# Scores of a gated linear attention on four quarters of TensorE, r and k scaled in one operation, score banks filled in bursts of two

## Chip, cores and metric

One core of one Trainium2 chip. The time is the device's, in microseconds, median of three runs.

## What is computed

Inputs r, k, v, w are [4, 8, 768, 48] (batch, head, token, feature), u is [8, 48]. The attention is a recurrence with a decay for each feature; its output, 3,072 rows of 384, goes through two feed-forward blocks.

```
for t in range(S):
    cur = einsum('bhd,bhe->bhde', u * k[t], v[t])
    y[t] = einsum('bhd,bhde->bhe', r[t], state + cur)
    state = w[t][..., None] * state + einsum('bhd,bhe->bhde', k[t], v[t])
h = maximum(maximum(x @ w1, x @ w2), x @ w3);  x = h @ w_out          # [3072, 384]
h = x @ w_in2;  solu = h * softmax(h);  ln = layernorm(solu) * g_ln;  out = ln @ w_out2
```

## The kernel before

**Groups and slots.** Tokens are cut into 6 units of 128. A group `g` is one unit of one batch element, 24 in all; its 8 heads lie in 4 pairs `q`, the first head of a pair on partitions 0 to 47 and the second on 64 to 111. Within a group the scores of token s against token t are made by levels, since the decay between two tokens is a product: level 0 takes a token with itself (with `u`), level 1 its neighbour, and the levels L = 2 to 64 take, in each block of 2L tokens, the late half (r) against the early half (k). Before each next level r of the late half and k of the early half are multiplied in place by products of w, a tree of products that GpSimd makes (`tree`, L411). A group has 8 such slots, `s` = 0 to 7, so 192 in all.

**One slot on each engine.** TensorE (`scores`, L439) makes 4 matmuls, one a pair, of 112 rows (both heads), 128 weight columns (tokens s) and 128 moving columns (2 heads x 64 tokens t). The heads are kept apart by `r_own`, which holds r twice, each time with zeros where the other head's features are. The result fills one PSUM bank. VectorE (`scores`, L700, and `scale`, L685) scales k (L696) and r (L698) for the next level, and for `s` up to 4 moves the slot's result through a mask to `scoresT` (L711, or L719 as a predicated copy). For `s` = 5 to 7 ScalarE copies blocks (L601). ScalarE's `base` (L576) makes `r_base` and `k_base` with `u` for slots 0 and 1 (L583 to L588).

**The mix** `M` of a group (TensorE, L462) turns k to tokens (L471), multiplies the carried state (L483, L484) and the values by the scores (L486), into columns 0 to 63 and 64 to 111 of the output, and makes the update of the state (L493). `v` is VectorE's new state, `q` and `p` split y and regroup it by DMA (`y_last` to `xT`).

**Feed-forward work.** `u` are 9 matmuls of 512 columns (L498 to L500), `d` the same, `l` 18, `t` 8 transposes (L552), `o` 8 fp32 matmuls of 384 columns, 16 records (L561). `e`, `x`, `c`, `n`, `w` are the softmax and norm on ScalarE and VectorE; `z` splits a chunk of weights.

**What sets the order.** Every engine walks the same list `PROGRAM`, put together from plans written out by hand (`START`, `FIRST`, `STEADY` four times, `LAST`); a dot stands for the next slot in `slot_order`, where slots 4 to 7 of a group alternate with slots 0 to 3 of the next, a digit for the next slot of that group. SP walks it too and issues the loads. The score banks are 4 and 5 (`LEV`), used in turn by slots and by the mix's turned k and update. TensorE waits in `wait_drained` for the reader of the bank's user two places back, so one slot's matmuls run while the other bank is read:

```
n = BANK_AT[user] - 2
kind, task = BANK_USERS[n]
...
if task[1] < 2 + MASKED:
    return masked, MASKED_AT["s", task]
return score_copied, COPIED_AT["s", task]
```

A slot also waits for the scaling of the slot before in its own group (`scaled`), VectorE's scaling for the end of that slot's matmuls (`scored`).

Of the kernel before, what the change touches and what calls it, by code (L numbers as in the profile page):

```python
# [22 lines left out]
UPDATES = 7  # L23
RING_K, RING_W, RING_P = 3, 2, 2
# [22 lines left out]
def splits(chunks, on_pool):  # L47
# [12 lines left out]
    . . . . u00 z u01 z u02 z u10 u11 u12 u20 u21 d0 . u22 d1 u30 d2 z . u31 . . M v z z . z u32 u40 u41 . u42 . d3 .  # L60
    u50 p . z u51 u52 . . d4 q d5 z M p . e0 v l0 g . x0 l1 q c0 . e1 t0 g . c1 x1 g . n00 g l2 . t1 n01 . e2 . n02 o0
    n03 M w0 e3 c2 v x2 l3 . w1 o1 . . t2 p . x3 . o2 n10 c3 q . . t3 . . M w2 p n11 n12 n13 q w3 o3 v"""

STEADY = """
    . . u00 . u01 . u02 u10 u11 d0 u12 . . u20 u21 . u22 . d1 v u30 u31 M d2 u32 . u40 u41 . . u42 u50 d3 . . u51 . .
    u52 d4 q . d5 M l0 v x0 . l1 . e0 c0 . t0 . e1 x1 . q c1 n00 o0 . . n01 t1 p . v M n02 w0 n03 . l2 p . q e2 x2 e3
    l3 c2 . o1 w1 t2 . . x3 p . n10 o2 c3 n11 t3 . p n12 w2 n13 . M q w3 v o3"""
# [63 lines left out]
COPIED_AT = places(lambda t: t[0] == "s" and t[1][1] >= 2 + MASKED)  # L131
UPDATED = places(lambda t: t[0] == "s" and t[1][1] >= 1)


def attention_moe_kernel(nc, r_in, k_in, w_in, v, u_in, w1, w2, w3, w_out, w_in2, w_out2, g_ln, base_mask, level_mask, ident_in, out):
# [3 lines left out]
    with ctx:  # L139
# [12 lines left out]
        base_m = sb("base_m", [128, 2, C // 2])  # L152
        level_m = sb("level_m", [128, MASKED, C // 2], u32)
        ident = sb("ident", [128, 128])

        r_own = sb("r_own", [128, RING_K, 2, PAIRS * C])
        k_sb = sb("k_sb", [128, RING_K, PAIRS * C])
# [5 lines left out]
        r_base = sb("r_base", [128, 2, PAIRS, C // 2])  # L163
        scoresT = sb("scoresT", [128, RING_P, PAIRS, 2, C])
# [25 lines left out]
        LEV = [4, 5]  # L190
        Y, OUT = 6, 7

        cleared = [sem(f"cleared{i}") for i in range(2)]
# [7 lines left out]
        kr_loaded = [sem(f"kr_loaded{i}") for i in range(RING_K)]  # L201
# [5 lines left out]
        k_scaled = sem("k_scaled")  # L207
# [84 lines left out]
        def logits_of(m, t):  # L292
# [3 lines left out]
        BANK_USERS = [("s", n) if kind == "s" else (part, n) for kind, n in PROGRAM  # L296
                      for part in (("s",) if kind == "s" else ("kt", "upd") if kind == "M" else ())] + [("after", 0), ("after", 1)]
        BANK_AT = {user: n for n, user in enumerate(BANK_USERS)}

        def bank_of(user):  # L300
            return LEV[BANK_AT[user] % 2]

        def drained(user):

            n = BANK_AT[user] - 2
            if n < 0:
                return None
            kind, task = BANK_USERS[n]
            if kind == "kt":
                return k_copied, task[0] + 1  # L310
            if kind == "upd":
                return state_new, task[0] + 1
            if task[1] < 2 + MASKED:
                return masked, MASKED_AT["s", task]
            return score_copied, COPIED_AT["s", task]

# [3 lines left out]
        def _(sp):  # L320
# [7 lines left out]
            def load_kr(g):  # L328
                slot = g % RING_K
                if g >= RING_K:  # L330
                    sp.wait_ge(y_done, g - RING_K + 1)
                    sp.wait_ge(k_turned, g - RING_K + 1)
                sp.dma_start(k_sb[0:PR, slot, :], k_in[g]).then_inc(kr_loaded[slot], 16)
                if g < RING_K:
                    sp.wait_ge(cleared[0], slot + 1)
                    sp.wait_ge(cleared[1], slot + 1)
                sp.dma_start(r_own[0:D, slot, 0, :], r_in[g, 0]).then_inc(kr_loaded[slot], 16)
                sp.dma_start(r_own[HB:PR, slot, 1, :], r_in[g, 1]).then_inc(kr_loaded[slot], 16)
# [67 lines left out]
        def _(pool):  # L406
            for i in range(RING_K):
                nc.gpsimd.memset(r_own[0:HB, i, 1, :], 0.0).then_inc(cleared[1], 1)
            nc.gpsimd.memset(state[:], 0.0).then_inc(cleared[1], 1)
# [22 lines left out]
        def _(pe):  # L432

            def wait_drained(user):
                before = drained(user)
                if before:
                    pe.wait_ge(before[0], before[1])

            def scores(g, s):  # L439
                slot = g % RING_K  # L440
                bank = ps[:, bank_of(("s", (g, s))), :]
                wait_drained(("s", (g, s)))
                if s == 0:
                    pe.wait_ge(r_base_done, g + 1)
                elif s == 1:
                    pe.wait_ge(k_base_done, g + 1)
                else:
                    pe.wait_ge(scaled, UPDATED["s", (g, s - 1)])
                for q in range(PAIRS):
                    cols = slice(q * C, (q + 1) * C)  # L450
                    r = r_own[0:PR, slot, :, cols]
                    if s == 0:
                        stationary, moving = k_sb[0:PR, slot, cols], r_base[0:PR, :, q, :]
                    elif s == 1:
                        stationary, moving = k_base[0:PR, cols], r.rearrange("p i (t e) -> p i t e", e=2)[:, :, :, 1]
                    else:
                        stationary = k_sb[0:PR, slot, cols]
                        moving = r.rearrange("p i (n h l) -> p i n h l", h=2, l=LEVELS[s - 2])[:, :, :, 1, :]
                    last = nc.tensor.matmul(bank[:, cols], stationary, moving, start=True, stop=True)  # L459
                last.then_inc(scored, 1)  # L460

            def mix(g):  # L462
                b, slot, p = g % B, g % RING_K, g % RING_P
                kt, upd, yp = ps[:, bank_of(("kt", (g,))), :], ps[:, bank_of(("upd", (g,))), :], ps[:, Y, :]
                wait_drained(("kt", (g,)))
                if g == 0:
                    pe.wait_ge(c_loaded, 16 * 3)
                    pe.wait_ge(cleared[1], RING_K + 1)
                pe.wait_ge(k_scaled, UPDATED["s", (g, SLOTS - 1)])
# [3 lines left out]
                pe.wait_ge(scaled, UPDATED["s", (g, SLOTS - 1)])  # L473
# [5 lines left out]
                if g >= B:  # L479
                    pe.wait_ge(state_new, g - B + 1)  # L480
                for q in range(PAIRS):
                    cols = slice(q * C, (q + 1) * C)
                    nc.tensor.matmul(yp[0:HB, cols], state[0:PR, b, q, 0:HB], r_own[0:PR, slot, 0, cols], start=True, stop=False)  # L483
                    nc.tensor.matmul(yp[HB:PR, cols], state[0:PR, b, q, 0:D], r_own[0:PR, slot, 1, cols], start=True, stop=False)  # L484
                    for i in range(2):
                        last = nc.tensor.matmul(yp[i * HB:i * HB + D, cols], v_sb[:, slot, (2 * q + i) * D:(2 * q + i + 1) * D],  # L486
                                                scoresT[:, p, q, i, :], start=False, stop=True)
                last.then_inc(y_done, 1)
                wait_drained(("upd", (g,)))
# [30 lines left out]
            def up(m, j, w):  # L520
                n = 3 * j + w
                if n == 0:
                    wait_split(3 * KD)
                    pe.wait_ge(repacked, B * REPACK * (m + 1))
                if n >= 2:
# [7 lines left out]
            def logits_(m, t):  # L533
# [4 lines left out]
                if m == UNITS - 1 and t == 2:  # L538
                    for before in map(drained, (("after", 0), ("after", 1))):
                        pe.wait_ge(before[0], before[1])  # L540
# [26 lines left out]
        def _(act):  # L567
# [8 lines left out]
            def base(g):  # L576
                slot = g % RING_K
                act.wait_ge(kr_loaded[slot], 48 * (g // RING_K + 1))
                if g:
                    act.wait_ge(scored, SCORED["s", (g - 1, 1)])  # L580
                r_even = r_own[0:PR, slot, :, :].rearrange("p i (q t e) -> p q i t e", q=PAIRS, e=2)[:, :, :, :, 0]
                for q in range(PAIRS):
                    last = nc.scalar.activation(r_base[0:PR, :, q, :], r_even[:, q, :, :], ACT.Copy, scale=u_sb[0:PR, q:q + 1])  # L583
# [7 lines left out]
            def scores(g, s):  # L591
# [3 lines left out]
                bank = ps[:, bank_of(("s", (g, s))), :].rearrange("p (a n l) -> p a n l", a=2 * PAIRS, l=L)  # L595
                dst = scoresT[:, g % RING_P, :, :, :].rearrange("p q i (n h l) -> p (q i) n h l", h=2, l=L)
                act.wait_ge(masked, MASKED_AT["s", (g, 1 + MASKED)])
                act.wait_ge(scored, SCORED["s", (g, s)])
                for n in range(C // (2 * L)):
                    early = slice(n * 2 * L, n * 2 * L + L)  # L600
                    last = nc.scalar.copy(dst[early, :, n, 1, :], bank[early, :, n, :])  # L601
                last.then_inc(score_copied, 1)

            def mix(g):
# [3 lines left out]
                nc.scalar.copy(k_tok[:].rearrange("p q d -> p (q d)"), ps[:, bank_of(("kt", (g,))), 0:PAIRS * PR]).then_inc(k_copied, 1)  # L608
# [71 lines left out]
        def _(dve):  # L680
            for i in range(RING_K):
                nc.vector.memset(r_own[0:PR, i, 0, :], 0.0).then_inc(cleared[0], 1)
            dve.wait_ge(c_loaded, 16 * 3)

            def scale(g, n):  # L685
# [3 lines left out]
                dv = decay_of(g, n).rearrange("p (n h) -> p n h", h=2)  # L689
# [5 lines left out]
                early = halves(k_sb[0:PR, slot, :], L)[:, :, 0, :]  # L695
# [157 lines left out]
```

## Time and profile before

| | |
|---|---|
| median of 3 runs | 858.72 us (857.13 to 861.47) |
| profiled execution | 861.66 us |
| its span | 859.9 us |
| mean granted TensorE clock | 0.99 |
| TensorE busy, records | 815.1 us, 5088 matmuls |
| VectorE / ScalarE / GpSimd busy | 473.9 / 331.4 / 76.2 us |
| first `u` of the six units | 91.5, 226.2, 361.3, 496.3, 631.4, 760.0 us |

An fp32 matmul shows as two records, each with its weight load (PEld). Records of matmuls overlap, since a record reaches to the end of the pipeline: the distance of starts is the pace, the duration is not. Forms such as `112*128 112x128` give weight rows x weight columns, then rows x moving columns. "Idle before" is the engine's idle time just before the instructions of a group.

### The profile page before, as it was taken

The page shows a single profiled execution, that of the slowest core. Times are in us where ns is not written, and L with a number is a line of the kernel's source. Part 1 is how long each engine was busy: PE and PEld are TensorE (multiplying, and loading weights), DVE is VectorE, ACT ScalarE, POOL GpSimd, SP SyncE. Part 2 cuts the span into 40 slices and gives each one's busy share as a digit, 9 for nine tenths or more (in the row PEclk, how much of TensorE's full clock was granted, in tenths as well). Part 3 has the DMA queues.
Part 4 walks back from the last instruction along what each step waited for, and adds up shares of the span by engine and source line. Part 5 has one row for each costly group of instructions (what it writes and reads, how often), then busy time and mean ns, then how long its engine had stood idle before and what let it go on. Part 6 is the DMA issues. An engine that isn't in the chain of part 4 may idle for free.

```text
span 859.9 us, 13390 instructions
## 1 busy us (share of the span) xinstructions
PE 815.1 (95%) x5088; PEld 669.9 (78%) x5088; DVE 473.9 (55%) x958; ACT 331.4 (39%) x741; POOL 76.2 (9%) x181
## 2 busy tenths in 40 slices
PE   5778999999999999999999999999999999999997
PEld 5667788887788887788887688887778888778774
DVE  4977556766543685544666544666644467412241
ACT  4444232566231365321463422344613235511153
POOL 3221111110010110100101101001101010000000
PEclk9988999999999999999999999999999999999999
DMA  8452201020101102201011011011020100000000
GB/s 221 123 170 62 65 26 53 6 83 26 63 1 40 44 8 63 62 3 41 1 45 55 20 57 42 1 45 55 15 63 1 41 6 11 19 23 1 1 10 27
DMA packets 27824, 36.50 MB, mean 42 GB/s; under 512 B 5232, under 2 KB 18160, under 8 KB 27760
## 3 DMA queue, kind: packets, MB, share of 16 engines
q1 hardware_dynamic: 27200, 35.41, 13.7%
q8 instruction: 41, 0.67, 0.3%
q10 hardware_dynamic: 560, 0.23, 0.1%
q14 instruction: 23, 0.19, 0.1%
HBM read 28.55 MB, written 4.72 MB: 39 GB/s over the span
## 4 chain that ended last, share of the span: by engine, by line
PE 87%; DVE 9%; issue 2%; ACT 1%; DMA 1%; SPq 0%; ACTq 0%; DVEq 0%
PE ps L459 19%; PE ps L498 16%; PE ps L500 15%; PE ps L499 15%; PE ps L561 14%; DVE r_own L698 3%; DVE scoresT L719 2%; PE ps L552 2%; PE ps L486 2%; PE ps L493 1%; DVE k_sb L696 1%; PE ps L484 1%; PE ps L471 1%; DVE scoresT L711 1%; PE ps L483 1%
## 5 line engine op out<-in xcount | busy, mean ns | idle before, releaser
L459 PE MATMUL ps<-r_own,k_sb 112*128 112x128 f32 x1152 | 159.2, 286 | 20.7 <-DVE r_own L698 11.8
L459 PEld LDWEIGHTS ps<-r_own,k_sb 112*128 112x128 f32 x1152 | 149.4, 198 | 33.1 <-issue 11.1
L498 PE MATMUL ps<-xT,w_moe 128*128 128x512 f32 x324 | 131.7, 406 | 1.5 <-DMA xT<-y_last 0.9
L561 PE MATMUL ps<-w_moe_out,zT 128*128 128x384 f32 x384 | 128.6, 488 | 3.9 <-ACT out_sb L674 2.6
L499 PE MATMUL ps<-xT,w_moe 128*128 128x512 f32 x324 | 127.9, 395 | 0.0
L500 PE MATMUL ps<-xT,w_moe 128*128 128x512 f32 x324 | 127.8, 395 | 0.0
L561 PEld LDWEIGHTS ps<-w_moe_out,zT 128*128 128x128 f32 x384 | 71.0, 190 | 50.0 <-issue 3.5
L698 DVE TENSOR_TENSOR r_own<-r_own,decay 112x512 f32<-112x512 f32 x144 | 103.2, 717 | 0.0
L696 DVE TENSOR_TENSOR k_sb<-k_sb,decay 112x256 f32<-112x256 f32 x144 | 62.6, 435 | 71.8 <-PE ps L459 71.5
L601 ACT COPY scoresT<-ps 16x128 f32<-16x128 f32 (+2 forms) x168 | 55.9, 333 | 95.9 <-PE ps L459 94.6
L639 ACT CAST h_x<-e_sb 128x512 fp32r<-128x512 f32 x36 | 22.3, 620 | 155.7 <-DVE e_sb L755 147.9
L498 PEld LDWEIGHTS ps<-xT,w_moe 128*128 128x128 f32 x324 | 61.1, 189 | 14.9 <-issue 1.4
L500 PEld LDWEIGHTS ps<-xT,w_moe 128*128 128x128 f32 x324 | 61.0, 188 | 14.3
L499 PEld LDWEIGHTS ps<-xT,w_moe 128*128 128x128 f32 x324 | 61.1, 189 | 12.3
L421 POOL TENSOR_TENSOR decay<-w_sb 112x256 f32<-112x256 f32 x24 | 15.4, 641 | 567.0 <-issue 537.1
L719 DVE COPY_PREDICATED scoresT<-level_m,ps 128x512 f32<-128x512 uint32 x72 | 65.0, 903 | 0.0
L498 PE MATMUL ps<-w_moe,h_x 128*128 128x512 f32 x144 | 58.8, 409 | 1.5 <-DVE h_x L764 1.5
L500 PE MATMUL ps<-w_moe,h_x 128*128 128x512 f32 x144 | 56.8, 395 | 0.0
L755 DVE TENSOR_TENSOR e_sb<-ps,e_sb 128x512 f32<-128x512 f32 x36 | 24.9, 691 | 57.8 <-PE ps L500 57.7
L499 PE MATMUL ps<-w_moe,h_x 128*128 128x512 f32 x144 | 56.8, 394 | 0.0
L749 DVE TENSOR_TENSOR e_sb<-ps,e_sb 128x512 f32<-128x512 f32 x36 | 24.9, 691 | 49.3 <-PE ps L500 49.3
L768 DVE TENSOR_REDUCE neg_max<-ps 128x1 f32<-128x1024 f32 x24 | 29.3, 1221 | 40.5 <-PE ps L500 40.5
(82 smaller groups left out, 1210.3 us busy)
## 6 DMA issues: line engine op xcount, KB each, us to landing
k_sb<-in_k SPq DMA_DIRECT2D x24, 224.0 KB, 2.7
w_sb<-in_w SPq DMA_DIRECT2D x24, 224.0 KB, 3.5
r_own<-in_r SPq DMA_DIRECT2D x48, 96.0 KB, 3.2
v_sb<-in_v SPq DMA_DIRECT2D x24, 192.0 KB, 3.7
out<-out_sb SPq DMA_DIRECT2D x24, 192.0 KB, 1.9
xT<-y_last SPq DMA_DIRECT2D x144, 16.0 KB, 1.9
e_sb<-in_w SPq DMA_DIRECT2D x5, 384.0 KB, 3.4
zT<-in_w SPq DMA_DIRECT2D x4, 384.0 KB, 5.4
```

The costliest lines, as they stand in the source:

```text
L459: last = nc.tensor.matmul(bank[:, cols], stationary, moving, start=True, stop=True)
L498: nc.tensor.matmul(o, a[0], b[0], start=first, stop=False)
L499: nc.tensor.matmul(o, a[0], b[1], start=False, stop=False)
L500: return nc.tensor.matmul(o, a[1], b[0], start=False, stop=last)
L561: last = nc.tensor.matmul(ps[:, OUT, 0:DM], zT[:, t % 2, c, :], w_moe2_out[:, c, :], start=(c == 0), stop=(c == J2 - 1))
L601: last = nc.scalar.copy(dst[early, :, n, 1, :], bank[early, :, n, :])
L696: nc.vector.tensor_tensor(early, early, dv[:, :, 1].unsqueeze(2).to_broadcast([PR, blocks, L]), ALU.mult).then_inc(k_scaled, 1)
L698: nc.vector.tensor_tensor(late, late, dv[:, :, 0].unsqueeze(1).unsqueeze(3).to_broadcast([PR, 2, blocks, L]), ALU.mult).then_inc(scaled, 1)
L719: nc.vector.copy_predicated(dst, mk, src).then_inc(masked, 1)
L749: nc.vector.tensor_tensor(c1, ps[:, (3 * j + 1) % 2, :], c1, ALU.max).then_inc(c2_done, 1)
L755: nc.vector.tensor_tensor(h_max, ps[:, (3 * j + 2) % 2, :], c1, ALU.max).then_inc(c3_done, 1)
L768: nc.vector.tensor_reduce(neg_max[:, t:t + 1], logits_of(m, t), AX.X, ALU.max, negate=True).then_inc(max_done, 1)
```

## The change

Scores go to four quarters of the array: `i`, the head, picks 48 rows, `h`, the half of the tokens, 64 weight columns. r is held once, beside k in `rk_sb`, loaded by one DMA. The head's result goes to a bank of its own, so a slot needs two banks and fills 128 columns of each, and two slots, a burst, fill the first half of both (`at` is the place). Up to two slots that follow each other on TensorE form a burst; its first slot waits for the readers of the last burst in these banks, and masks and copies wait for the burst's last matmul. Before the first `u`, bursts alternate between banks 4, 5 and 0, 1 (`EARLY`). One operation scales r and k. A mask is two operations, one for each half of the tokens. `r_base` is made for one copy of r. The state's products use one head's 48 rows each and stand ahead of all products with the values. The plans `START`, `FIRST` and `STEADY` are new, `LAST` is not.

```diff
-    b0 0 a0 0 a1 0 z 1 1 0 1 0 a2 z 0 1 0 1 z 0 z 1 b1 z M z v p q 1 2 2 1 2 z b2 v M a3 z 3 p 2 q 2 z 2 3 2 2 3 M b3 v
-    q b4 3 3 a4 3 p 4 3 4 3 4 a5 M v q 4 p b5"""
+    0 a0 0 1 0 1 a1 0 z b0 1 0 z a2 0 1 b1 0 1 z 0 1 z v M q p 1 2 1 2 z 2 b2 a3 b3 z M v p z z 3 2 2 3 z q 2 a4 3 2 3
+    2 M v p b4 q 3 4 3 p 4 3 4 3 M v q a5 4 b5"""
...
+    . . u00 . . u01 u02 u10 u11 u12 . . u20 v u21 M d0 . u22 u30 u31 d1 . . d2 u32 u40 u41 . d3 u42 . u50 . . u51 u52 .
+    d4 q d5 M v l0 . x0 e0 . p q c0 l1 . p . e1 t0 . . o0 x1 . . n00 p n01 n02 c1 l2 n03 v t1 M o1 w0 q . w1 x2 e2 . c2
+    l3 . t2 . e3 . x3 c3 n10 o2 . n11 . . t3 w2 n12 M n13 q v o3 p w3 . ."""
...
+def bursts():
+
+    found, begun = [], False
+    for n, (kind, task) in enumerate(t for t in PROGRAM if t[0] in "sMudlto"):
+        begun = begun or kind == "u"
+        if kind == "s":
+            if found and found[-1][0][-1][0] == n - 1 and len(found[-1][0]) < 2:
+                found[-1][0].append((n, task))
+            else:
+                found.append(([(n, task)], begun))
+    return [([task for _, task in slots], begun) for slots, begun in found]
...
+                BANK_USERS["s", n] = LEV if n % 2 == 0 or BURSTS[n][1] else EARLY
...
-                wait_drained(("s", (g, s)))
+                banks, at, begins = banks_of(g, s)
+                if begins:
+                    wait_drained(("s", BURST_OF[g, s][0]))
...
-                    last = nc.tensor.matmul(bank[:, cols], stationary, moving, start=True, stop=True)
+                    for h in range(2 if s < SLOTS - 1 else 1):
+                        for i, rows in enumerate((slice(0, D), slice(HB, PR))):
+                            early = slice(q * C + h * HALF, q * C + (h + 1) * HALF)
...
+                                stationary, moving, width = k_sb[rows, slot, early], r_sb[rows, slot, q * C + HALF:(q + 1) * C], HALF
+                            last = nc.tensor.matmul(ps[h * HALF:(h + 1) * HALF, banks[i], at + q * width:at + (q + 1) * width],
+                                                    stationary, moving, start=True, stop=True)
...
-                    nc.tensor.matmul(yp[0:HB, cols], state[0:PR, b, q, 0:HB], r_own[0:PR, slot, 0, cols], start=True, stop=False)
-                    nc.tensor.matmul(yp[HB:PR, cols], state[0:PR, b, q, 0:D], r_own[0:PR, slot, 1, cols], start=True, stop=False)
+                    for i, rows in enumerate((HB, D)):
+                        part = slice(i * HB, i * HB + D)
+                        nc.tensor.matmul(yp[i * HB:i * HB + rows, cols], state[part, b, q, 0:rows], r_sb[part, slot, cols],
+                                         start=q == 0, stop=False, skip_group_check=True)
...
-                nc.vector.tensor_tensor(early, early, dv[:, :, 1].unsqueeze(2).to_broadcast([PR, blocks, L]), ALU.mult).then_inc(k_scaled, 1)
-                late = r_own[0:PR, slot, :, :].rearrange("p i (n h l) -> p i n h l", h=2, l=L)[:, :, :, 1, :]
-                nc.vector.tensor_tensor(late, late, dv[:, :, 0].unsqueeze(1).unsqueeze(3).to_broadcast([PR, 2, blocks, L]), ALU.mult).then_inc(scaled, 1)
+                row = rk_sb[0:PR, slot, :, :]
+                both = bass.AP(row.tensor, row.offset + L, [row.ap[0], [PAIRS * C - L, 2], [2 * L, blocks], [1, L]])
+                by = decay_of(g, n).rearrange("p (n h) -> p h n", h=2).unsqueeze(3).to_broadcast([PR, 2, blocks, L])
+                nc.vector.tensor_tensor(both, both, by, ALU.mult).then_inc(scaled, 1)
...
+                for h in range(2):
+                    rows = slice(h * HALF, (h + 1) * HALF)
+                    src, dst = score_views(g, s, rows)
```

## Rows read from the trace of the kernel before

**Rows 1.** The page: busy time of each engine; the chain by engine.

```profile
PE 815.1 (95%) x5088; PEld 669.9 (78%) x5088; DVE 473.9 (55%) x958; ACT 331.4 (39%) x741; POOL 76.2 (9%) x181
...
PE 87%; DVE 9%; issue 2%; ACT 1%; DMA 1%; SPq 0%; ACTq 0%; DVEq 0%
```

**Rows 2.** Busy time by stretch: stretch, length, engines, clock, DMA share, GB/s.

```profile
0.00:91.40 91.40, 65.97 (x527) 60.38 (x528) 67.59 (x120) 37.69 (x106) 20.71 (x50) 0.91 0.49 141
91.40:226.10 134.70, 131.52 (x834) 107.81 (x834) 79.97 (x158) 60.90 (x135) 18.52 (x33) 1.00 0.13 40
226.10:361.20 135.10, 132.68 (x851) 109.47 (x850) 76.39 (x158) 52.37 (x119) 10.55 (x28) 1.00 0.12 35
...
631.30:759.90 128.60, 127.12 (x803) 104.00 (x801) 68.96 (x146) 47.48 (x101) 5.36 (x14) 1.00 0.08 22
```

**Rows 3.** TensorE's waits, first 91.4 us: total, times, longest.

```profile
PE ps L459 <- DVE r_own L698: 11.8, 8, 1.9
```

**Rows 4.** Timeline of TensorE, two slots: start, length, records.

```profile
304.34 1.05 PE L459 MATMUL ps<-r_base,k_sb 112*128 112x128 f32 x8
305.24 1.06 PE L459 MATMUL ps<-r_own,k_sb 112*128 112x128 f32 x8
```

**Rows 5.** Timeline of TensorE, state products of a mix.

```profile
319.33 0.27 PE L484 MATMUL ps<-r_own,state 112*48 112x128 f32 x1
319.34 0.27 PE L483 MATMUL ps<-r_own,state 112*64 112x128 f32 x1
319.44 0.27 PE L484 MATMUL ps<-r_own,state 112*48 112x128 f32 x1
```

**Rows 6.** Its update and the score behind it; the update's group by form.

```profile
320.75 0.67 PE L493 MATMUL ps<-v_sb,k_tok 128*64 128x48 f32 x16
321.35 0.38 PE L459 MATMUL ps<-r_own,k_sb 112*128 112x128 f32 x1
...
L493 PE MATMUL ps<-v_sb,k_tok 128*64 128x48 f32 x192 | 15.4, 223 | 4.6 <-DVE scoresT L719 4.1 <-ACT k_tok L608 0.4
```

**Rows 7.** Timeline of TensorE from the transposes to the state products.

```profile
318.37 0.55 PE L471 MATMUL ps<-ident,k_sb 112*128 112x112 f32 x4
...
318.66 0.26 PE L471 MATMUL ps<-ident,k_sb 112*128 112x112 f32 x1
...
318.85 0.32 PE L483 MATMUL ps<-r_own,state 112*64 112x128 f32 x1
...
319.01 0.27 PE L483 MATMUL ps<-r_own,state 112*64 112x128 f32 x1
```

**Rows 8.** Timeline of TensorE, full-width matmuls behind another update.

```profile
189.07 0.50 PE L498 MATMUL ps<-w_moe,h_x 128*128 128x512 f32 x1
189.40 0.39 PE L499 MATMUL ps<-w_moe,h_x 128*128 128x512 f32 x1
189.63 0.39 PE L500 MATMUL ps<-w_moe,h_x 128*128 128x512 f32 x1
```

**Rows 9.** Timeline of VectorE, two stretches: scaling and masks.

```profile
30.62 0.43 DVE L696 TENSOR_TENSOR k_sb<-k_sb,decay 112x256 f32<-112x256 f32 x1 [0.21 <-PE ps L459]
30.96 0.68 DVE L698 TENSOR_TENSOR r_own<-r_own,decay 112x512 f32<-112x512 f32 x1
31.57 0.69 DVE L719 COPY_PREDICATED scoresT<-level_m,ps 128x512 f32<-128x512 uint32 x1
32.16 0.95 DVE L743 TENSOR_TENSOR w_moe<-zT,w_moe 128x768 fp32r<-128x768 f32 x1
...
121.70 1.31 DVE L719 COPY_PREDICATED scoresT<-level_m,ps 128x512 f32<-128x512 uint32 x1
```

**Rows 10.** ScalarE's `r_base` by form: busy us, mean ns, idle before.

```profile
L583 ACT ACTIVATE r_base<-r_own,u_sb 112x128 f32<-112x128 f32 x96 | 31.4, 399 | 11.4 <-PE ps L459 7.1 <-DMA r_own<-in_r 3.9
```

**Rows 11.** DMA issues: KB each, us to landing.

```profile
r_own<-in_r SPq DMA_DIRECT2D x48, 96.0 KB, 3.2
```

**Rows 12.** TensorE's group of scores from 91.4 us on, by form.

```profile
L459 PE MATMUL ps<-r_own,k_sb 112*128 112x128 f32 x928 | 121.4, 276 | 5.3 <-DVE scoresT L719 2.8 <-DVE scoresT L711 2.5
```

More of the change, by code:

```diff
@@ L190, in attention_moe_kernel @@
         LEV = [4, 5]
+        EARLY = [0, 1]
         Y, OUT = 6, 7
-        cleared = [sem(f"cleared{i}") for i in range(2)]
+        cleared = sem("cleared")
         u_loaded = sem("u_loaded")
@@ L200, in attention_moe_kernel @@
         wg_ready = sem("wg_ready")
[L201 removed]
+        rk_loaded = [sem(f"rk_loaded{i}") for i in range(RING_K)]
         v_loaded = [sem(f"v_loaded{i}") for i in range(RING_K)]
@@ L293, in logits_of @@
             return ps[:, pair_of(m, t):pair_of(m, t) + 2, :].rearrange("p a n -> p (a n)")
[L296 to L301, printed above, removed]
-        def drained(user):
[L305 to L315, printed above, removed]
+        BANK_USERS = {}
@@ new lines, in attention_moe_kernel @@
+        for kind, task in PROGRAM:
+            if kind == "s" and BURST_OF[task][1] == 0:
+                n = BURST_OF[task][0]
+                BANK_USERS["s", n] = LEV if n % 2 == 0 or BURSTS[n][1] else EARLY
+            elif kind == "M":
+                BANK_USERS["kt", task[0]] = LEV[:1]
+                BANK_USERS["upd", task[0]] = LEV[1:]
+            elif kind == "u" and task in ((0, 0, 0), (0, 0, 1)):
+                BANK_USERS[kind, task[2]] = EARLY[task[2]:task[2] + 1]
+        BANK_USERS["after", 0] = LEV
@@ new lines, in drained, with banks_of @@
+        def drained(user):
+            users = list(BANK_USERS)
+            before = users[:users.index(user)]
+            found = {}
+            for bank in BANK_USERS[user]:
+                for other in [o for o in before if bank in BANK_USERS[o]][-1:]:
+                    for signal, value in read_out(other):
+                        found[signal.name] = (signal, value)
+            return list(found.values())
+        def banks_of(g, s):
+            n, place = BURST_OF[g, s]
+            return BANK_USERS["s", n], place * 2 * C, place == 0
@@ new lines, in score_views, with score_ready @@
+        def score_views(g, s, rows):
+            banks, at, _ = banks_of(g, s)
+            width = HALF if s == SLOTS - 1 else HALF // 2
+            src = ps[rows, banks[0]:banks[0] + 2, at:at + PAIRS * width].rearrange("p i (q t) -> p i q t", t=width)
+            return src, scoresT[rows, g % RING_P, :, :, :]
+        def score_ready(g, s, engine):
+            n, place = BURST_OF[g, s]
+            slots = BURSTS[n][0]
+            other = [t for t in slots[:place] if (t[1] < 2 + MASKED) != engine]
+            return SCORED["s", slots[-1]], other[-1:]
@@ L332, in load_kr @@
                     sp.wait_ge(k_turned, g - RING_K + 1)
[L333 to L338, printed above, removed]
+                sp.dma_start(rk_sb[0:PR, slot, :, :], rk_in[g]).then_inc(rk_loaded[slot], 16)
             def load_v(g):
@@ L406, in _ @@
         def _(pool):
-            for i in range(RING_K):
-                nc.gpsimd.memset(r_own[0:HB, i, 1, :], 0.0).then_inc(cleared[1], 1)
-            nc.gpsimd.memset(state[:], 0.0).then_inc(cleared[1], 1)
+            nc.gpsimd.memset(state[:], 0.0).then_inc(cleared, 1)
             def tree(g):
@@ L538, in logits_ @@
                 if m == UNITS - 1 and t == 2:
-                    for before in map(drained, (("after", 0), ("after", 1))):
-                        pe.wait_ge(before[0], before[1])
+                    wait_drained(("after", 0))
                 for n in range(2):
@@ L680, in _ @@
         def _(dve):
-            for i in range(RING_K):
-                nc.vector.memset(r_own[0:PR, i, 0, :], 0.0).then_inc(cleared[0], 1)
+            nc.vector.memset(scoresT[HB:128, :, :, :, 0:HALF], 0.0).then_inc(cleared, 1)
             dve.wait_ge(c_loaded, 16 * 3)
@@ L721, in y_low @@
+                last.then_inc(masked, 1)
             def y_low(g):
```

157 lines of the change are left out of this document (88 added, 69 removed).

## The prediction

> **What bounds the kernel now.** I read the page's busy shares and its chain of waits first. TensorE is busy for 95% of the span and holds 87% of the chain; VectorE holds 9% of it at 55% busy [rows 1]. Then the stretches: in the first 91 us TensorE is busy for only 66 of 91.4 us at a mean clock of 0.91, and VectorE for 68 [rows 2]. From 91.4 to 760 us TensorE idles for 2.4 to 3.2 us in each unit of some 135 us, and 1.5 in the last of them (length less busy time, [rows 2]). So there are two regimes: a start bound by the dependent steps between TensorE and VectorE, where the scores' matmuls wait 11.8 us on the scaling of `r_own` alone [rows 3], and a rest in which TensorE's own work is the time.
>
> **What a slot costs.** The 192 slots are 4 fp32 matmuls each, which the trace shows as 8 records; two slots start 0.90 us apart, so 0.112 us a record [rows 4]. Of the 192, 40 stand ahead of the first `u` in `START` and 152 behind it.
>
> **Part 1: scores on quarters.** A slot becomes 16 matmuls (8 for the last level), 32 records, with 64 weight columns and 32 moving columns (64 in the last level). No row shows a matmul on 48 rows of one half. The nearest rows are the ones that already use column halves. The state products on output columns 0 to 63 and 64 to 111 start 10 ns apart, and the next pair 0.11 us later [rows 5]: the column halves run side by side, each at the pace that a full-width record has. The update's 16 records of 48 moving and 64 or 48 weight columns take 0.67 us; less the 0.22 us of the last one, the eighth of a half starts 0.45 us after the first, 0.064 us a record, a first delayed one among them [rows 6]. That is a little over half of 0.112 for half the weight columns, though the moving columns fell to 48: loading weights sets the pace. I take 0.06 us a record. With four quarters side by side, each has 8 records a slot (4 pairs, two records each): 8 x 0.06 = 0.48 us; in the last level two quarters have 8 records each, again 0.48. The bounds: if only column halves overlap, 16 x 0.06 = 0.96 (if all parts share the pace of the update's 16 records in 0.45 us, 32 x 0.028 = 0.90); if a record costs its 32 moving columns alone, a quarter of 0.112, 8 x 0.028 = 0.22. I take 0.48, since a quarter's records have the update's weight columns. After `START` that is 152 x (0.90 - 0.48) = 63 us less.
>
> The Trainium skill, TensorEngine Tiling (Array Packing), Instruction Overhead, speaks against this: it gives each matmul some 60 cycles of overhead and says not to tile a dimension that is already small. At 2.4 GHz that would be, as an estimate from that page, 25 ns for each of 32 records or 0.8 us a slot, and part 1 would shrink to 15 us. By that page the change would gain nothing here; what it says hangs on whether parts share the overhead, and the 10 ns between two column halves [rows 5] speak against that.
>
> **Part 2: changing the array's division.** Each run of slots between other work now goes from whole array to quarters and back. The trace shows both ways, where the mix does it. Into halves: the last of four transposes starts at 318.66 (the first at 318.37, so 0.096 apart), the first state product at 318.85, 0.19 later, so +0.09; its second pair comes 0.15 us later where 0.11 is the rule, +0.04 [rows 7]. Back: the last update record starts at 321.20 and the next score at 321.35, +0.09 over a pace of 0.06; and the second full-width matmul behind such a change comes 0.33 us after the first, where 0.23 is the rule, +0.10 [rows 6, 8]: its weights were not loaded ahead. Together 0.33 us a round. I counted the new plans: 85 runs of slots behind `START` that are not joined to a mix, so 28 us, and the mix, which now goes from quarters (state products) to column halves (values), one more change of 0.09 in 20 groups, 2 us. Sum +30. Bounds for a round: 0.10, if weights can be loaded ahead after all, and 0.50.
>
> **Part 3: VectorE.** The scaling of k (0.43 us) disappears and r and k, 512 elements a partition as `r_own` had, take one operation. Back to back, operations start 0.34 us (256 elements) and 0.61 us (512) after each other [rows 9]. A mask becomes two operations of 64 partitions and 256 elements: 2 x 0.34 for 0.59 to 0.61, +0.08; the first level, at 1.31 where the next ones take 0.69 [rows 9], perhaps +0.15. After `START` VectorE has room: 80 of 135 us busy [rows 2]. In `START` it is on the path: 34 scalings less 0.34 each are 11.6 us, 26 masks give 2 back, and the slots' shorter matmuls are mostly eaten by the coarser waits of part 4. I take -9 us. ScalarE's `r_base` halves its elements, from 399 ns [rows 10] to less, off the path. r comes with k in one transfer of 448 KB for three of 416 KB in all, of which r's took 3.2 us each [rows 11], asked for a group or more ahead; SP issues two fewer a group and no longer waits for the zeroed `r_own`, and the first load may land some tenths of a us later or earlier. Nothing.
>
> **Part 4: one set of banks.** Before, a slot waited for the one two places earlier; now both slots of a burst fill both banks, and a burst waits until VectorE and ScalarE have read both slots of the last one. Behind the waiting matmul the whole of TensorE queues. After a burst ends VectorE owes the second slot's scaling (0.61) and four mask operations (4 x 0.34), with a hop of 0.1 some 2.1 us. One `u` between bursts (9 x 0.23 = 2.1 us, [rows 8]) covers that. I walked the new order for places with less cover behind `START`: 8 where two bursts adjoin, 11 with only a set of transposes (0.88 us) between. 8 x 2.1 + 11 x 1.2 = 30 us. Of today's waits of scores behind `START`, 5.3 us [rows 12], these take the place: +25.
>
> **Sum.** -63 + 30 - 9 + 25 = -17 us. The profiled execution took 861.7 us (span 859.9), 3 us over the median of 858.7 of the runs shown; 861.7 - 17 = 845 for a profiled one, and 842 for the median.
>
> **Rivals.**
> A, the quarters don't run side by side, so that the change doesn't do what it says: the row halves share what loads weights, or all quarters share one pace of records. No row has two row halves at once. A slot then takes 0.90 to 0.96 us; at 0.96 the 152 slots add 9 instead of taking 63, the changes keep their 30, `START` gains only some 5, and the uncovered places shrink to perhaps +10, as VectorE works under longer slots: 859 + 9 + 30 - 5 + 10 = 903 us, at 0.90 some 894. It decides the sign from about 0.60 us a slot on. For it: the update's pace is set by weights. Against it: column halves load side by side [rows 5], and rows of the array are fed by partitions of their own. The Trainium skill, TensorEngine Tiling, Key Properties, says that different tiles load and multiply in parallel; no row of this case shows it for row halves. Chance 0.12, all slower.
> B, the single set of banks eats the gain. If the need after a burst is 3.0 us, not 2.1 (masks on half the partitions at nearly their old 0.69, the first level at 1.3 twice), the 19 places add 0.9 each, 17 us, and places covered by one `u` begin to wait. 859 to 866 us. For it: VectorE's waits already lead in `START` [rows 3]. Against it: 256 elements take 0.34 us back to back, 0.43 alone [rows 9]. Chance 0.14, of which 0.10 within the bound and 0.04 slower.
> C, changing the division costs 0.10 a round, since another quarter's weights can be loaded while one runs: 85 x 0.23 = 20 us less, 822 us. Against it: two changes that each show theirs [rows 6 to 8]. Chance 0.10, faster.
> D, TensorE works so little in the start that its clock falls. It is at 0.91 there already with 66 of 91 us busy [rows 2], and the change takes off some 16 us of that work. At half clock a slot of 0.48 takes 0.96; if 30 of the 40 do, and half of it shows, 7 us: 849. Chance 0.04, faster.
>
> **Numbers.** The forecast itself gets 0.60, between 830 and 853 us: 0.58 faster, 0.01 no change and 0.01 slower. A measurement of this kernel tells 0.5%, 4.3 us, from no change. Faster: 0.58 + 0.10 + 0.04 = 0.72. Same: 0.01 + 0.10 = 0.11. Slower: 0.01 + 0.12 + 0.04 = 0.17. The range, 814 to 867, holds the forecast, B, D and all but the end of C, and leaves out A and what lies under C: about 0.16.
>
> **What would show it.** Right: a slot of `L459`'s successor spans about 0.48 us and two slots under 1.1; 64-column records of one quarter start 0.06 us apart and four quarters within 0.03; the first full-width matmul after a burst shows a gap of about 0.1 to the next; waits of scores on VectorE's masks of some 2 us, four a unit; a unit of about 133 us where 135.1 stood; the first `u` at about 82 us, not 91. Wrong: records one after the other at 0.028 or more (A), a unit over 135 us with waits at places that have a `u` between (B), no gap at the changes (C), PEclk under 0.8 before 80 us (D).

## The result and the profile after

The changed kernel takes 861.43 us against 858.07 in runs side by side, a ratio of 1.0034 (95% interval 1.0020 to 1.0049): 0.3% slower where 1.9% faster was forecast. (One of its 20 executions took 2567 us, and one of the ten of run h1 below 4246 us; both are left out of the ratios.) The time lies near the upper end of the range of 814 to 867, on the other side of the kernel before.

The page of the changed kernel, busy time, the granted clock over the span in tenths (40 slices) and the chain by engine:

```profile
span 861.4 us, 21718 instructions
PE 785.2 (91%) x9312; PEld 611.7 (71%) x9312; DVE 440.3 (51%) x908; ACT 325.2 (38%) x741; POOL 68.8 (8%) x178
...
PEclk9956899979999999899999899998989999999999
...
PE 79%; DVE 10%; issue 5%; ACT 3%; DMA 1%; SPq 1%; DVEq 0%; ACTq 0%
```

TensorE is busy for 30 us less than in [rows 1] and VectorE for 34 us less, and still the span is longer. The stretches from the first `u` of a unit to the next, as in [rows 2] (length; PE, PEld, DVE, ACT, POOL busy; clock; DMA share; GB/s), and all five units together:

```profile
0.00:87.90 87.90, 54.03 (x1392) 48.35 (x1392) 60.77 (x111) 35.90 (x105) 17.53 (x47) 0.79 0.49 141
87.90:232.20 144.30, 131.83 (x1585) 100.96 (x1585) 75.84 (x154) 60.80 (x136) 17.50 (x33) 0.95 0.16 47
232.20:368.30 136.10, 129.06 (x1556) 99.81 (x1552) 71.18 (x150) 51.22 (x119) 9.68 (x28) 0.95 0.14 41
...
87.90:762.90 675.00, 640.15 (x7536) 494.10 (x7537) 351.21 (x733) 260.64 (x594) 51.30 (x131) 0.96 0.13 36
```

The clock stood at 1.00 in every stretch behind `START` before, and at 0.91 in `START`; now it is 0.95 in a unit and 0.79 in `START`. The first unit behind `START` is 9.6 us longer than before (144.3 against 134.7), the other four together 3 us shorter. Next, TensorE's timeline, two slots between full-width matmuls, which answers to [rows 4, 7, 8]:

```profile
301.31 0.39 PE L558 MATMUL ps<-w_moe,h_x 128*128 128x512 f32 x1
301.63 0.67 PE L512 MATMUL ps<-rk_sb 48*64 48x32 f32 x32
302.12 0.65 PE L512 MATMUL ps<-r_base,rk_sb 48*64 48x32 f32 x32
302.70 0.50 PE L556 MATMUL ps<-w_moe,h_x 128*128 128x512 f32 x1
303.03 0.39 PE L557 MATMUL ps<-w_moe,h_x 128*128 128x512 f32 x1
```

A slot is 32 records in 0.49 us, 15 ns a record. The quarters run side by side: in this slot the first records of all four start within 20 ns, the next four come 79 ns later, and all further ones 58 ns behind the four ahead of them. Into the quarters costs 0.32 where 0.23 is the pace, out of them 0.58 where 0.49 is, and the second full-width matmul behind them comes after 0.33 where 0.23 is the pace. And the place where two bursts adjoin:

```profile
227.96 0.67 PE L512 MATMUL ps<-rk_sb 48*64 48x32 f32 x32
228.45 0.65 PE L512 MATMUL ps<-r_base,rk_sb 48*64 48x32 f32 x32
231.10 0.67 PE L512 MATMUL ps<-rk_sb 48*64 48x32 f32 x32 [2.01 <-DVE scoresT L779]
231.59 0.65 PE L512 MATMUL ps<-rk_sb,k_base 48*64 48x32 f32 x32
232.17 0.50 PE L556 MATMUL ps<-xT,w_moe 128*128 128x512 f32 x1
232.50 0.47 PE L557 MATMUL ps<-xT,w_moe 128*128 128x512 f32 x1
232.77 0.63 PE L558 MATMUL ps<-xT,w_moe 128*128 128x512 f32 x1
233.20 0.63 PE L556 MATMUL ps<-xT,w_moe 128*128 128x512 f32 x1
233.62 0.63 PE L557 MATMUL ps<-xT,w_moe 128*128 128x512 f32 x1
```

The wait for the masks is 2.01 us, as forecast. But behind it the 512-column matmuls start 0.43 us apart, not 0.23. The stretches around it show why:

```profile
228.00:232.70 4.70, 2.69 (x131) 2.49 (x131) 3.15 (x7) 0.91 (x3) 0.00 (x0) 1.00 0.59 174
232.70:236.10 3.40, 3.40 (x16) 2.19 (x18) 1.29 (x3) 0.81 (x4) 0.00 (x0) 0.50 0.47 155
236.10:240.00 3.90, 3.90 (x77) 3.35 (x74) 3.20 (x5) 3.22 (x11) 0.00 (x0) 1.00 0.00 2
```

The granted clock falls to its lower level (1.2 GHz) for 3.4 us, right behind 4.7 us in which TensorE ran four thin slots and stood idle for 2. This happens at 10 places behind `START`, 54 us in all, where before there was none, the last microsecond of the span apart. In `START` it is 36 us against 17, and the last of these stretches reaches 5 us into the first unit.

### The profile page after: what moved, and what is told of

Its sections match the earlier page's. It is cut to its first block, busy times and chain, and to the rows that moved or that the text cites. A ratio compares the mean times of both kernels' runs of the same rounds, so it can differ in the third digit from the quotient of the medians.

```text
span 861.4 us, 21718 instructions
## 1 busy us (share of the span) xinstructions
PE 785.2 (91%) x9312; PEld 611.7 (71%) x9312; DVE 440.3 (51%) x908; ACT 325.2 (38%) x741; POOL 68.8 (8%) x178
## 4 chain that ended last, share of the span: by engine, by line
PE 79%; DVE 10%; issue 5%; ACT 3%; DMA 1%; SPq 1%; DVEq 0%; ACTq 0%
PE ps L556 16%; PE ps L620 14%; PE ps L558 14%; PE ps L557 14%; PE ps L512 10%; PE ps L539 3%; PE ps L544 3%; DVE scoresT L786 3%; DVE rk_sb L758 3%; DVE scoresT L779 2%; PE ps L525 2%; PE ps L611 1%; ACT scoresT L663 1%; DVE e_sb L842 1%; PE ps L551 1%
## 5 line engine op out<-in xcount | busy, mean ns | idle before, releaser
L512 PE MATMUL ps<-rk_sb 48*64 48x32 f32 (+1 forms) x4224 | 100.4, 235 | 46.8 <-DVE rk_sb L758 21.7
L758 DVE TENSOR_TENSOR rk_sb<-rk_sb,decay 112x512 f32<-112x512 f32 x144 | 98.2, 696 | 87.2 <-PE ps L512 86.3
L512 PEld LDWEIGHTS ps<-rk_sb 48*64 48x64 f32 x4224 | 88.0, 150 | 76.9 <-issue 32.7
L620 PE MATMUL ps<-w_moe_out,zT 128*128 128x384 f32 x384 | 136.8, 512 | 3.6 <-ACT out_sb L736 2.2
L556 PE MATMUL ps<-xT,w_moe 128*128 128x512 f32 x324 | 132.9, 410 | 1.4 <-DMA xT<-y_last 1.4
L558 PE MATMUL ps<-xT,w_moe 128*128 128x512 f32 x324 | 129.4, 399 | 0.0
L557 PE MATMUL ps<-xT,w_moe 128*128 128x512 f32 x324 | 129.2, 399 | 0.0
L620 PEld LDWEIGHTS ps<-w_moe_out,zT 128*128 128x128 f32 x384 | 74.4, 199 | 53.9 <-issue 9.5
L786 DVE COPY_PREDICATED scoresT<-level_m,ps 64x256 f32<-64x256 uint32 x144 | 76.3, 530 | 5.9 <-PE ps L512 2.9
L556 PEld LDWEIGHTS ps<-xT,w_moe 128*128 128x128 f32 x324 | 62.3, 192 | 15.9 <-issue 2.1
L558 PEld LDWEIGHTS ps<-xT,w_moe 128*128 128x128 f32 x324 | 62.5, 193 | 13.7
L557 PEld LDWEIGHTS ps<-xT,w_moe 128*128 128x128 f32 x324 | 62.6, 193 | 12.2
L469 POOL TENSOR_TENSOR decay<-w_sb 112x256 f32<-112x256 f32 x24 | 18.1, 754 | 596.7 <-issue 539.4
L779 DVE TENSOR_TENSOR scoresT<-ps,base_m 64x256 f32<-64x256 f32 x96 | 40.5, 422 | 29.1 <-PE ps L512 18.8
```

Source lines behind the costliest of these rows:

```text
L512: last = nc.tensor.matmul(ps[h * HALF:(h + 1) * HALF, banks[i], at + q * width:at + (q + 1) * width], stationary, moving, start=True, stop ...
L556: nc.tensor.matmul(o, a[0], b[0], start=first, stop=False)
L557: nc.tensor.matmul(o, a[0], b[1], start=False, stop=False)
L558: return nc.tensor.matmul(o, a[1], b[0], start=False, stop=last)
L620: last = nc.tensor.matmul(ps[:, OUT, 0:DM], zT[:, t % 2, c, :], w_moe2_out[:, c, :], start=(c == 0), stop=(c == J2 - 1))
L758: nc.vector.tensor_tensor(both, both, by, ALU.mult).then_inc(scaled, 1)
```

## The experiments

Theory T1: the forecast terms are right, and what is missing is the clock. T2: a term is wrong in size, and the clock falls where TensorE waits anyway. "Half clock" is the time at a granted clock of 0.5.

**b0, the kernel before.** No edit.

> The kernel before, unchanged, for a trace from the same chip as the runs beside it. Both theories: span 860 us within 3, clock 0.99. The 512-column matmuls started 232 ns apart in the trace of before and 227 ns apart in that of the changed kernel: if that is the chip's, they are 227 ns apart here too; if it is the change's (where tensors lie, or what runs beside), 232.

Measured: 859.3 us in one execution, span 857.5; the 512-column matmuls start 232 ns apart, so the pace is not the chip's. The first `u` comes at 89.0, not 91.5: that much `START` varies from one execution of the same kernel to the next.

**f1, the waits behind START filled.**

```diff
+FILL = {(6, 4): (7, 8), (7, 1): (7, 8)}
+for g in range(8, GROUPS, 4):
+    FILL[g, 5] = 0, 7
+    if g > 8:
+        FILL[g, 3] = 0, 7
+for g in range(10, GROUPS, 4):
+    FILL[g, 6] = 7, 5
...
                 banks, at, begins = banks_of(g, s)
+                bank, n = FILL.get((g, s), (0, 0))
+                for _ in range(n):
+                    nc.tensor.matmul(ps[:, bank, :], w_moe1[:, 0, 0, 0:128], w_moe1[:, 0, 1, 0:512], start=True, stop=True)
```

> The changed kernel with idle TensorE time filled at 14 places behind START by 5 to 8 dummy 512-column matmuls each (into banks 0 and 7 while nobody uses them), no longer than the waits that stand there. Nothing of the computation changes. Theory T1, the granted clock: the waits themselves were forecast rightly, and what was lost is the clock that falls to half at each of them (54 us at half clock behind START). Then the clock behind START is 1.00 throughout, the waits' ends stay where they are, and the time falls by 15 to 25 us, to 838 to 846. Theory T2, TensorE was waiting anyway in those stretches or a term of the sum was wrong in size, and the clock costs little: no change, 858 to 866.

Measured: 846.0 us, ratio to before 0.9861 (0.9831 to 0.9891), against 1.0034 for the change alone: 15 us. (The places are 13; the expectation miscounted.) T1 holds behind `START` and T2 falls there: work that computes nothing, put into waits, makes the kernel faster. Half clock behind `START` went from 54 to 7 us; what is left came behind two waits of 1.1 and 1.2 us in the first unit that were not filled. Its second unit, to be held against 136.10 above and 135.10 in [rows 2]:

```profile
232.60:362.90 130.30, 128.03 (x1579) 98.97 (x1571) 71.12 (x150) 51.23 (x119) 9.70 (x28) 1.00 0.15 43
```

What f1 gives back lies in the last four units and not in the first. The four together in the changed kernel, then f1's first unit (144.30 above) and its four:

```profile
232.20:762.90 530.70, 508.32 (x5956) 393.13 (x5953) 275.36 (x580) 199.84 (x458) 33.80 (x98) 0.96 0.12 33
...
88.80:232.60 143.80, 136.10 (x1607) 103.87 (x1607) 75.35 (x154) 60.66 (x136) 17.98 (x33) 0.96 0.16 47
232.60:745.80 513.20, 504.28 (x6023) 389.51 (x6015) 275.79 (x580) 200.07 (x458) 33.78 (x98) 1.00 0.12 34
```

**f2, the waits of START filled**, with `nc.tensor.matmul(ps[:, 2, 0:128], ident[:], ident[:], ...)`, 1 to 9 times at 12 slots and ahead of two mixes.

> The changed kernel with dummy fp32 matmuls of ident (into bank 2) in the waits between the first mix and the first u only. T1: half clock in START goes from 41 us to under 15, the first u comes at 80 to 84 us, not 88, and the time falls by 4 to 8 us. T2: START hangs on VectorE whatever the clock, first u at 88, no change.

Measured: 858.8 us, ratio 1.0009 (0.9988 to 1.0030), so 2 us less than the change, but the two intervals overlap; first `u` at 86.1. Half clock in `START` fell from 36 to 7 us. That is T1's direction, but less than its 4 to 8 us and later than its 80 to 84: with the clock up, `START` is still only 3 us shorter than b0's. The clock was not all that `START` lost.

**f12, both.**

> f1 and f2 together: dummy matmuls in the long waits of START and behind it. The two act on different stretches, so by T1 they add: f1's 846.0 less the 2.6 us that f2 took, some 843 to 845, half clock under 16 us in all. If VectorE sets START alone, 846.

Measured: 845.4 us, ratio 0.9846 (0.9817 to 0.9874); against f1 the difference is within the noise of both.

**o1, the order alone.** `START`, `FIRST` and `STEADY` of the changed kernel in the kernel before.

> The kernel before with the changed kernel's plans START, FIRST and STEADY, and nothing else of the change: the order alone. The new order puts slots side by side that wait for each other, so with 0.90 us a slot and two banks used in turn it should cost some: 861 to 872 us. If the order brought a gain by itself, under 856.

Measured: 870.3 us, ratio 1.0147 (1.0109 to 1.0186), as expected: with full-width slots the new order costs some 12 us. In the profiled execution 7 of them are in the first unit, the plan `FIRST` (134.7 before), with the clock at 1.00:

```profile
88.00:229.60 141.60, 134.60 (x857) 110.77 (x857) 80.97 (x162) 61.70 (x138) 18.27 (x33) 1.00 0.15 47
```

**o2, full-width slots with the waits of one set of banks.**

```diff
                 wait_drained(("s", (g, s)))
+                if BURST_OF[g, s][1] == 0:
+                    last = drained(("s", (g, s)), 1)
+                    if last:
+                        pe.wait_ge(last[0], last[1])
```

> o1 (kernel before with the new plans, full-width slots) in which the first slot of each burst also waits for the reader of the slot just ahead, as the single set of banks makes it do. So it has idle stretches of some 1 to 2 us at the same places, but slots of 0.90 us of the whole array around them. Theory T1a, the idle time alone makes the clock fall: half clock behind START of 20 us or more, 885 to 900. Theory T1b, it takes idle time together with thin quarter slots: clock stays 1.00 behind START, and the time is o1's 870 and the waits, 875 to 885.

Measured: 913.5 us, ratio 1.0647. Both expectations of the time miss, since the waits cost more than I reckoned, above all in `START` (first `u` at 117, not 88). What tells T1a from T1b is the clock behind `START`, and there it is T1b: half clock for 3.4 us in all, against 54. Idle time of 1.5 to 1.7 us, three slots of 0.9 us around it, the clock at 1.00 for the unit:

```profile
387.88 1.13 PE L479 MATMUL ps<-r_own,k_sb 112*128 112x128 f32 x8 [1.70 <-ACT scoresT L621]
402.65 1.13 PE L479 MATMUL ps<-r_own,k_sb 112*128 112x128 f32 x8 [1.47 <-DVE scoresT L731]
...
265.70:404.40 138.70, 132.77 (x850) 109.54 (x849) 76.18 (x158) 52.09 (x119) 10.08 (x28) 1.00 0.13 39
```

The waits in this unit are shorter than the changed kernel's 2.0 and 2.4 us, though. So h2 gave the thin slots waits of about the same length. In o2's first unit there are also waits as long as the changed kernel's, and the clock is 1.00 there too:

```profile
194.85 1.13 PE L479 MATMUL ps<-r_own,k_sb 112*128 112x128 f32 x8 [2.09 <-issue]
218.63 1.13 PE L479 MATMUL ps<-r_own,k_sb 112*128 112x128 f32 x8 [2.01 <-DVE r_own L718]
...
117.20:265.70 148.50, 135.63 (x859) 110.75 (x858) 81.29 (x163) 62.49 (x139) 18.86 (x33) 1.00 0.13 39
```

Full width alone does not keep the clock up, though. In o2's `START`, where 16 waits of 1.2 to 2.7 us stand within 117 us, it is 0.79:

```profile
0.00:117.20 117.20, 74.21 (x521) 68.40 (x521) 66.72 (x118) 37.46 (x104) 18.04 (x50) 0.79 0.36 109
```

**h2, fewer dummies.** In f1, `FILL[g, 5] = 0, 2` and `FILL[g, 3] = 0, 3`.

> f1 with 2 or 3 full-width dummies at those 7 places instead of 7, so that some 1.2 to 1.6 us of idle time are left there, about what o2 had with full-width slots and a clock of 1.00. If idle time alone decides, the clock stays up as in o2: 846. If thin slots around it count too (T1b), half clock comes back at some of the places: 849 to 856.

Measured: 856.7 us, ratio 0.9987 (0.9965 to 1.0009), a little over T1b's. Half clock behind `START` is 27 us where f1 had 7. It comes behind four of the seven waits, which are 1.35 to 1.49 us long, no longer than o2's; the first of these two is one of them (half clock from 351.5 on), the second is not:

```profile
351.13 0.82 PE L523 MATMUL ps<-rk_sb 48*64 48x32 f32 x32 [1.49 <-DVE scoresT L797]
365.82 0.67 PE L523 MATMUL ps<-rk_sb 48*64 48x32 f32 x32 [1.35 <-DVE scoresT L790]
...
234.70:366.90 132.20, 128.91 (x1567) 99.41 (x1563) 70.95 (x150) 51.18 (x119) 9.66 (x28) 0.97 0.15 43
```

So idle time alone does not decide; the thin slots around it count. They do not decide by themselves either: behind three of the seven waits the clock stayed up.

**h1, thin dummies.**

```diff
-    FILL[g, 5] = 0, 7
-    if g > 8:
-        FILL[g, 3] = 0, 7
+    THIN[g, 5] = 16
+    if g > 8:
+        THIN[g, 3] = 18
...
+                for _ in range(THIN.get((g, s), 0)):
+                    for h in range(2):
+                        for i, rows in enumerate((slice(0, D), slice(HB, PR))):
+                            nc.tensor.matmul(ps[h * HALF:(h + 1) * HALF, i, 0:32], w_moe1[rows, 0, 0, 0:HALF].bitcast(f32),
+                                             w_moe1[rows, 0, 1, 0:32].bitcast(f32), start=True, stop=True)
```

> f1 with the dummies at the adjoining bursts (7 places) made thin: not 7 full-width 512-column matmuls but 16 or 18 rounds of four quarter matmuls of 32 columns, which keep TensorE issuing for as long. Theory T1c, any records keep the clock up: no half clock there, 846. Theory T1d, what counts is how much of the array is at work: half clock comes back at about those 7 places, 3 to 7 us each, and the time rises to 852 to 858.

Measured: 859.8 us, ratio 1.0022 (1.0000 to 1.0045): T1d, and somewhat beyond. Half clock behind `START` is 41 us. The four microseconds up to the end of one such wait, filled with thin matmuls, and what follows:

```profile
346.50:350.50 4.00, 3.69 (x211) 3.56 (x204) 3.63 (x10) 2.77 (x10) 0.28 (x1) 1.00 0.02 4
350.50:357.30 6.80, 6.32 (x53) 5.29 (x52) 2.70 (x9) 2.15 (x4) 2.24 (x7) 0.50 0.09 31
```

TensorE was busy for 3.69 of 4.00 us, and the clock fell to half for 6.8 us. At the same wait in f1, with full-width dummies, it was busy for less, and the clock stayed (1.00 in f1's unit above):

```profile
344.20:348.20 4.00, 3.42 (x88) 2.69 (x84) 3.50 (x9) 3.06 (x12) 0.00 (x0) 1.00 0.01 2
```

At other places of h1 TensorE also stood idle for 1.2 us for a reason that the profile doesn't name, so its time is a little beyond what the clock alone explains. The dummies of h1 differ from f1's in more than one way (48 of 128 rows and 64 of 128 weight columns, 32 moving columns for 512, another type), and which of these counts was not tried.

**p1, the addresses of the kernel before.** f1 with unused tensors where the change made one smaller (`base_m`, `level_m`, r beside k, `r_base`), so that all later tensors lie as before.

```diff
+        pad_a = sb("pad_a", [128, HALF])
...
+        pad_c = sb("pad_c", [128, RING_K, PAIRS * C])
```

> f1 with four unused tensors where the change made a tensor smaller, so that all later ones (v_sb, xT, h_x2, e_sb and so on) lie at the addresses of the kernel before. The 512-column matmuls start 227 ns apart in all traces of the changed kernel and 232 in all of the kernel before. If that is where the operands lie, they go back to 232 here and the time rises by 1728 x 4.8 ns = 8 us over f1, to 854. If it is something else that the change did, 227 and 846.

Measured: 853.0 us, ratio 0.9941 (0.9920 to 0.9962), 7 us over f1, and the 512-column matmuls start 232 ns apart again.

**l1, the addresses of the changed kernel in the kernel before**, for the tensors of the feed-forward work. `k_sb` and `r_base` declared last, a pad of 384 bytes a partition.

> The kernel before with k_sb and r_base declared last and a pad of 384 bytes a partition, so that xT, h_x2, e_sb and zT lie at the addresses of the changed kernel. By p1's result the 512-column matmuls start 227 ns apart, and the time falls by 8 us to 850. If the pace hangs on something else that the pads of p1 touched, 232 and 858.

Measured: 850.0 us, ratio 0.9922 (0.9896 to 0.9947), 227 ns. A move of declarations is worth 7 us to the kernel before (8 by the medians), and the change had brought it along unnoticed.

**s1, r and k scaled in two operations.** In f1:

```diff
-                nc.vector.tensor_tensor(both, both, by, ALU.mult).then_inc(scaled, 1)
+                for a, side in ((k_sb, 0), (r_sb, 1)):
+                    part = halves(a[0:PR, slot, :], L)[:, :, side, :]
+                    last = nc.vector.tensor_tensor(part, part, dv[:, :, 1 - side].unsqueeze(2).to_broadcast([PR, blocks, L]), ALU.mult)
+                last.then_inc(scaled, 1)
```

> f1 with r and k scaled in two operations of 256 elements again, not in one of 512. The prediction had the one operation worth 0.34 us a level: then START is 11 us longer and the time 855 or more. New theory: in the changed kernel's trace the one takes 0.66 to 0.72 us start to start where two of 256 would take 2 x 0.34, so the joined operation brought nothing: 845 to 848, first u within 1 us of f1's.

Measured: 853.7 us, ratio 0.9952 (0.9933 to 0.9970), 8 us over f1. My theory that the joined operation brings nothing falls. Where the 8 us are is less clear. The profiled executions differ by 5.8 us: the first `u` is at 91.8, 3.0 later, and the other 3 are in the units, where I had put nothing. But other kernels with f1's `START` have the first `u` at 87.9 (the change) to 90.8 (h2), so the 3.0 is hardly more than `START` varies; the prediction's 11 us there were too many. Two levels in s1:

```profile
26.95 1.43 DVE L772 TENSOR_TENSOR rk_sb<-rk_sb,decay 112x256 f32<-112x256 f32 x4
28.41 0.88 DVE L801 COPY_PREDICATED scoresT<-level_m,ps 64x256 f32<-64x256 uint32 x2
```

Four operations take 1.46 us, 0.73 a level, where the joined ones take 0.67 and k and r took 0.95 before. So most of what VectorE saves on scaling comes from r being held once, little from the joining, and why the joining is worth 8 us of time stays open.

**r1, two bursts parted.** f12 with `u00 . . u01 . . u02` for `. . u00 . . u01 u02` at the head of `STEADY`, and no dummies there.

> f12 with the first of the two adjoining bursts of each unit parted: STEADY begins with u00 and has each of its first two bursts one u later. No dummies there any more. The wait of 2.0 us goes at 4 places, if xT's regrouping by DMA has landed 2 us earlier than it was needed; 8 us less than f12, 834 to 839. If the DMA is what u00 then waits for, the wait only changes its name: no gain over f12.

Measured: 842.0 us, ratio 0.9812 (0.9783 to 0.9840), the lowest of all, 3 us under f12 and not 8, and the two intervals overlap. The wait of 2.0 us on the masks is gone, but `u00` now waits for the regrouping of y:

```profile
PE ps L571 <- DMA xT<-y_last: 5.5, 5, 2.5
```

## Why the prediction was wrong

The terms, all by the profiled executions (span 859.9 before, 861.4 after):

| term | forecast | measured |
|---|---|---|
| slots behind `START` | -63 (0.48 us each) | -62 (0.49 each, 152 x 0.41) |
| changes of the array's division | +30 (0.33 a round) | +26 (0.09 + 0.09 + 0.10 a round, 85 of them, and 2 for the mix as forecast) |
| waits behind `START` | +25 | +23 (idle 675.0 - 640.2 = 34.9, was 668.5 - 656.6 = 11.9); 9 of them in the first unit |
| `START` | -9 | about 0 (first `u` at 87.9 to 90.8 in the change, f1, h1, h2; 91.5 and 89.0 before) |
| clock behind `START` | 0 | +26 (what is left of a stretch longer by 6.5 us) |
| operands' addresses | not seen | -7 (p1), some of it behind the last unit |

The clock's 26 is a remainder: 6.5 + 62 - 26 - 23 + the 6 or so of the addresses that fall in the stretch.

**Parts 1, 2 and 4 were right.** The quarters run side by side, a record every 58 ns in each (rival A falls: 0.49 us a slot, not 0.90). Loading weights sets that pace: in the last level the records have 64 moving columns for 32, and the last of a slot's records starts 0.44 us after the first there, 0.45 in the other levels. The Trainium skill, TensorEngine Tiling (Array Packing), Key Properties, says that tiles load and multiply in parallel; the trace agrees, for row halves too, since four quarters start within 20 ns. The 60 cycles of overhead a matmul that the same page of the Trainium skill gives under Instruction Overhead are not paid one after the other by the quarters, which start 7 ns apart here. The single set of banks costs in sum what the walk of the order gave (rival B falls), and the change of division shows its price at every burst (rival C falls).

**The step that failed is the clock, rival D.** The sum has no term for it behind `START`, and the runs show some 26 us there. It was there with its mechanism, "TensorE works so little that its clock falls", but put into `START` alone, at 7 us and a chance of 0.04. Part 4 priced a wait of 2 us at 2 us. f1 shows that filling 13 waits gives 15 us back (18 in the profiled executions); the accounting of the stretch makes the whole of it some 26, and 54 us at half the clock would be 27 if TensorE worked all through. I took idle time for the thing to watch. h1 shows that it isn't alone: TensorE kept issuing thin matmuls, and the clock fell. h2 against o2 shows the same from the other side: with full-width slots around them, waits of 1.5 to 2.1 us behind `START` left the clock up, but for one of 1.7 us. What about the thin slots does it is not shown. So the very edit that saved 62 us made the waits beside it dear. The clock of 0.91 in `START` at 66 of 91 us busy [rows 2] was the hint, and I read it for `START` only. The sign that the prediction names for D, PEclk under 0.8 before 80 us, is there too: the third and fourth slices of the page above, of 21.5 us each, have 5 and 6.

**Part 3 was over-valued.** For `START` I took the joined scaling at -0.34 us and a mask at +0.08. The changed kernel's VectorE, in a stretch like [rows 9]:

```profile
26.38 1.29 DVE L758 TENSOR_TENSOR rk_sb<-rk_sb,decay 112x512 f32<-112x512 f32 x2
27.71 0.87 DVE L786 COPY_PREDICATED scoresT<-level_m,ps 64x256 f32<-64x256 uint32 x2
28.61 0.96 DVE L811 TENSOR_TENSOR w_moe<-zT,w_moe 128x768 fp32r<-128x768 f32 x1
```

The scaling takes 1.33 / 2 = 0.67 where k and r took 0.34 + 0.61 = 0.95, so -0.28. But the mask's two halves take 0.90 where one operation took 0.59, so +0.31: 34 x 0.28 less 26 x 0.31 is -1.5 us, not -9. That fits what f2 left; the masks were not tried by themselves, so their part is argued, not shown. With the clock up behind `START` and the addresses as before (p1), 5 us are left of the 17 that were forecast; this term is most of what is missing there.

**The addresses hid 7 us of the loss.** Held against l1, the kernel before with the same addresses, the change costs some 10 us (1.0034 against 0.9922). That the time lies within the stated range at all is luck: without these 7 us, which the forecast did not know of, it would be some 868.

**The first unit gains nothing.** It is 9.6 us longer than before, and f1 leaves it so (143.8). TensorE is idle for 12.5 us of it, 3.2 before. o1, with the new order and full-width slots, is 7 us longer there at a clock of 1.00, so the order has a part in it; the rest is not taken apart. The other four units of f1 are 21 us shorter than before (513.2 against 533.8), 5 of them by the addresses as l1 has them. The new plans with the old `FIRST` were not tried.

## What to carry over

Matmuls on quarters of the array do run side by side, but beside them waits of 1.1 to 2.5 us were followed, not always, by 3 to 10 us at half clock: price them so, fill them with full-width matmuls, or part the dependent bursts. Before a change is judged, compare the pace of an untouched matmul in both traces; if it moved, operands may have moved in memory, and that can be had without the change. And compare a new order unit by unit: here one of five lost nearly half of what the others gained.

## What the runs showed of the hardware that I had not expected

- Dummy full-width matmuls in waits: 861.4 to 846.0 us. Seven of the 13 filled with thin ones instead: 859.8.
- 512-column matmuls with 128 weight columns start 227 or 232 ns apart, by where tensors lie in on-chip memory and nothing else that differs (f1 and p1). 1728 of them make some 8 us; p1 and l1 measured 7. Which operand it is and by what rule was not tried.
- A predicated copy of 512 elements in runs of two takes 1.31 us, in longer runs 0.69 [rows 9]; two of 256 on half the partitions take 0.90, one of 512 on all 0.59, start to start.
- Changing the array's division costs some 0.3 us a round, most of the saving of one slot in quarters (0.41 us): runs of slots pay, single ones hardly do.
